# Layer two's first matrix product by Strassen's scheme, in a fused kernel of attention and two feed-forward layers

## Chip, cores and metric

The kernel runs on one core of one Trainium2 chip. The metric is the device time of one execution in microseconds, the median over runs; the profile is of one more execution of the same program.

## Reference

Attention over two batches of eight heads, 768 positions and 64 features each, in a window of 128 positions with four sink positions, then two feed-forward layers over the 1536 tokens of 512 features. The second layer, cut to what matters:

```python
n_tokens, d_model, d_ff = (1536, 512, 2048)

def _moe_ref(x, w_in, w_out):      # layer one
    h = x @ w_in
    g = np.maximum(0.01 * h, h)
    return (g @ w_out).astype(np.float32)

def _moe2_ref(x, w_in, w_out):     # layer two
    h = x @ w_in
    g = h * (1.0 / (1.0 + np.exp(-h)))
    return (g @ w_out).astype(np.float32)
```

## The kernel before

Every float32 operand of a matmul is split into a high part (rounded by ScalarE's copy into the type fp32r) and a low part (VectorE's subtraction of the high part from the whole); each product is three passes, high by high, high by low, low by high (`PASSES`). In the layers, the 2048 hidden features are 16 slices of 128 (`FT`), the tokens three blocks of 512 (`NB`), and a step `F` is one slice of one block of one layer: 96 steps, `steps` at its head. A step is two parts on PE. `hidden` multiplies a slice of w_in (`win`, four pieces of 128x128 along the 512 input features) by the block of x into the bank `h_ps`: 4 x 3 matmuls 512 wide, L805. `project` multiplies the slice of w_out by the hidden activations `g` into the four banks `y_ps`: again 12, L831. In layer two g is the stationary operand, so that y comes out with tokens on the partitions.

Between them, ACT takes `h_ps` twice (`take_hidden`, L466 into `g_f32`, L468 into the high part of `g`), and DVE makes the low part (`low_g`, L608). PE does hidden(F + 1) before project(F), which gives them the length of one part. Slices of weights come by DMA from SP's queue (`load_w`, L256) into a ring of four raw slots (`w_raw`, w_in and w_out of a slice side by side), and are split by ACT and DVE (`high_win` L453, `low_win` L597, `high_wout` L459, `low_wout` L603) into eight slots, `KEPT`. The tables `win_in` and `wout_in` say at which step. Blocks go through the slices in alternating directions, and the last eight of a block stay for the next, so 64 splits serve 96 steps. At the end of a block, `evacuate` brings `y_ps` out: in layer one as high and low part straight into `x` (L476, L618), in layer two into `out_sb`, from where SP stores it.

Attention runs ahead of layer one and beside it: its ticks `a` are woven into the steps up to F = 33. POOL works for attention alone: low parts of q, k and v (L330, L336, L345), of the attention's output (`low_x`, L315), and small copies (L306, L359). All engines run a program written out by hand, each in its own order, and wait for each other by semaphores. The order of PE for the steps behind attention is:

```python
for F in range(LAST - FS, NSTEP):
    if F + 1 < NSTEP:
        hidden(F + 1, 0)
        hidden(F + 1, 1)
    project(F, 0)
    project(F, 1)
```

Of the kernel before, what the change touches and what calls it, by code (L numbers as in the profile page):

```python
# [1 line left out]

# [9 lines left out]
P = 128  # L12
# [4 lines left out]
def sink_window_attention_two_ffn(  # L17
# [23 lines left out]
    KEPT = 8  # L41
# [4 lines left out]
    steps = [(layer, b, FT - 1 - i if b % 2 else i) for layer in (0, 1) for b in range(NB) for i in range(FT)]  # L46
    NSTEP = len(steps)
    N_L0 = FT * NB
# [4 lines left out]
    for F, (layer, b, f) in enumerate(steps):  # L53
        if (layer, f) not in resident:
            slot, left = free.pop(0)
            resident[layer, f] = len(split_w)
            split_w.append((layer, f))
            split_slot.append(slot)
            slot_left.append(left)
            first_step.append(F)  # L60
        j = resident[layer, f]
        split_of.append(j)
        if F % FT < FT - KEPT or b == NB - 1:
            del resident[layer, f]
            free.append((split_slot[j], F))
    NSPLIT = len(split_w)

# [8 lines left out]
    for j, s in enumerate(first_step):  # L76
        was, was_out = at, at_out
        start, i = s - s % FT, s % FT
# [36 lines left out]
    with ExitStack() as ctx:  # L115
# [9 lines left out]
        w_raw = sb("w_raw", [P, RING, 2 * HD], F32)  # L125
        win = sb("win", [P, KEPT, 2, HD], F32R)
        wout = sb("wout", [P, KEPT, 2, HD], F32R)

        x = sb("x", [P, 2, C, TILES * P], F32R)
        g_f32 = sb("g_f32", [P, 2, BLK], F32)  # L130
        g = sb("g", [P, 2, 2, BLK], F32R)

        qk_raw = sb("qk_raw", [P, 2, H // 2, QW], F32)
        v_raw = sb("v_raw", [P, HD], F32)
# [22 lines left out]
        filler = sb("filler", [P, 2 * P], BF16)  # L157
        out_sb = qk_raw[:, :, :, :].rearrange("p a b c -> p (a b c)")[:, 0:TB * HD].rearrange(
# [22 lines left out]
        def tokens(F):  # L181
            b = steps[F][1]
            return slice(b * BLK, (b + 1) * BLK)

# [31 lines left out]
        y_high, y_ready = sem("y_high"), sem("y_ready")  # L216
# [23 lines left out]
        def _(sp):  # L240
# [52 lines left out]
        def _(pool):  # L293
# [93 lines left out]

            for u in range(LAST):
# [545 lines left out]
```

## Time and profile before

| | |
|---|---|
| median of 3 runs | 667.64 us (667.15 to 668.63) |
| the profiled execution's own time | 668.03 us |
| its span, first to last instruction | 666.1 us |
| PE / ACT / DVE / POOL busy in the span | 638.8 / 299.9 / 278.7 / 120.0 us |
| mean granted clock of TensorE | 0.992 |
| read from HBM | 49.55 MB |

Span and busy times are of one execution. PE's busy time is that of its matmuls, which overlap: one lasts 0.39 us and the next starts before its end, so what a matmul costs is read from the distance of two starts. PEld is the load of the stationary operand, beside it. A group's "idle before" is time in which its engine stood before its instructions, with what ended that.

### The profile page before, as it was taken

Reading aid. Unit: us, or ns where it says so; the run is one execution under the profiler, and the core shown is the slowest. Engines: PE = TensorE matmul, PEld = TensorE weight load, DVE = VectorE, ACT = ScalarE, POOL = GpSimd, SP = SyncE. Lnnn points to the kernel's source line nnn. Section 1 sums busy time; section 2 is a strip of 40 time slices with the busy share of each in tenths; the row PEclk is TensorE's granted clock in tenths of the full one; section 3 lists DMA queues with packets and bytes.
Section 4 is the critical chain, followed back from the end, with each engine's and each line's share of the span. In section 5 each row is a group of like instructions: output and inputs, shape, how many; then the busy total and the mean of one; then the engine's idle time right before and its main releaser. Section 6 shows DMA issues by size and latency. Waiting matters only on the chain.

```text
span 666.1 us, 9036 instructions
## 1 busy us (share of the span) xinstructions
PE 638.8 (96%) x3091; PEld 526.7 (79%) x3091; DVE 278.7 (42%) x646; ACT 299.9 (45%) x676; POOL 120.0 (18%) x165
## 2 busy tenths in 40 slices
PE   8886999999989999999999999999999999999997
PEld 4675787777868888887888888888888888888886
DVE  3897456555535655543222234333322222212222
ACT  4787556555545565543333344333323333223332
POOL 5786324232314333310000000000000000000000
PEclk8999999999989999999999999999999999999999
DMA  6565233433322123111011123223211212201201
GB/s 148 147 189 161 64 112 96 132 107 112 95 81 64 49 64 112 64 33 31 1 63 64 64 68 110 98 101 99 95 64 31 64 63 64 96 0 64 63 1 63
DMA packets 16941, 53.27 MB, mean 80 GB/s; under 512 B 2561, under 2 KB 2561, under 8 KB 16897
## 3 DMA queue, kind: packets, MB, share of 16 engines
q1 hardware_dynamic: 16512, 52.63, 25.7%
q8 instruction: 25, 0.41, 0.3%
q14 instruction: 20, 0.16, 0.1%
q10 hardware_dynamic: 384, 0.07, 0.1%
HBM read 49.55 MB, written 3.15 MB: 79 GB/s over the span
## 4 chain that ended last, share of the span: by engine, by line
PE 77%; issue 9%; DVE 5%; ACT 4%; POOL 3%; DMA 2%; SPq 0%; POOLq 0%; ACTq 0%; DVEq 0%
PE h_ps L805 37%; PE y_ps L831 33%; PE o_ps L771 2%; DMA qk_raw<-qk 2%; PE s_ps L726 1%; ACT prob L416 1%; PE t_ps L739 1%; DVE win L597 1%; DVE wout L603 1%; DVE att L591 1%; ACT wout L459 1%; POOL k_hl L336 1%; DVE g L608 1%; ACT q_st L427 1%; POOL x L315 1%
## 5 line engine op out<-in xcount | busy, mean ns | idle before, releaser
L805 PE MATMUL h_ps<-x,win 128*128 128x512 f32 x1152 | 284.4, 394 | 9.4 <-DVE win L597 5.2
L805 PEld LDWEIGHTS h_ps<-x,win 128*128 128x128 f32 x1152 | 214.0, 189 | 54.2 <-DVE win L597 6.8
L466 ACT ACTIVATE g_f<-h_ps 128x512 f32<-128x512 f32 x96 | 57.4, 598 | 269.8 <-PE h_ps L805 269.6
L831 PE MATMUL y_ps<-g,wout 128*128 128x512 f32 x576 | 146.5, 395 | 1.2 <-PE o_ps L771 1.2
L831 PE MATMUL y_ps<-wout,g 128*128 128x512 f32 x576 | 138.2, 390 | 0.0
L603 DVE TENSOR_TENSOR wout<-w_raw,wout 128x512 fp32r<-128x512 f32 x64 | 46.7, 729 | 192.0 <-ACT wout L459 192.0
L831 PEld LDWEIGHTS y_ps<-wout,g 128*128 128x128 f32 x576 | 108.2, 188 | 22.4
L831 PEld LDWEIGHTS y_ps<-g,wout 128*128 128x128 f32 x576 | 104.0, 188 | 20.6 <-issue 1.9
L608 DVE TENSOR_TENSOR g<-g_f,g 128x512 fp32r<-128x512 f32 x96 | 66.1, 689 | 99.4 <-ACT g L468 99.4
L416 ACT ACTIVATE prob<-sm,neg_max 128x260 f32<-128x260 f32 (+1 forms) x96 | 47.0, 490 | 52.7 <-DVE neg_max L546 52.6
L468 ACT ACTIVATE g<-h_ps 128x512 fp32r<-128x512 f32 x96 | 57.0, 593 | 0.0
L597 DVE TENSOR_TENSOR win<-w_raw,win 128x512 fp32r<-128x512 f32 x64 | 49.1, 767 | 2.3 <-ACT win L453 2.3
L546 DVE CUSTOM_DVE_ANT_0 sm<-s_ps,mask 128x260 f32<-128x260 f32 (+1 forms) x71 | 28.7, 405 | 41.8 <-PE s_ps L726 41.1
L459 ACT ACTIVATE wout<-w_raw 128x512 fp32r<-128x512 f32 x64 | 40.4, 631 | 0.0
L453 ACT ACTIVATE win<-w_raw 128x512 fp32r<-128x512 f32 x64 | 40.3, 630 | 0.0
L330 POOL TENSOR_TENSOR q_st<-qk_raw,q_st 64x512 fp32r<-64x512 f32 x24 | 31.5, 1312 | 41.8 <-ACT q_st L427 40.2
L345 POOL TENSOR_TENSOR v_hl<-v_raw,v_hl 128x256 fp32r<-128x256 f32 x24 | 20.0, 834 | 100.6 <-ACT v_hl L435 100.5
L726 PEld LDWEIGHTS s_ps<-k_hl,q_st 128*128 128x128 f32 x142 | 26.9, 195 | 11.9 <-issue 3.5
L726 PE MATMUL s_ps<-k_hl,q_st 128*128 128x260 f32 (+1 forms) x142 | 30.2, 295 | 5.1 <-DVE neg_max L546 4.0
L771 PE MATMUL o_ps<-pT,v_hl 128*128 128x256 f32 x222 | 34.3, 288 | 0.1
L336 POOL TENSOR_TENSOR k_hl<-qk_raw,k_hl 128x528 fp32r<-128x528 f32 x22 | 31.1, 1413 | 1.7
L771 PEld LDWEIGHTS o_ps<-pT,v_hl 128*128 128x128 f32 x222 | 29.7, 191 | 0.7 <-DVE pT L554 0.4
(76 smaller groups left out, 407.4 us busy)
## 6 DMA issues: line engine op xcount, KB each, us to landing
w_raw<-w SPq DMA_DIRECT2D x64, 512.0 KB, 3.3
qk_raw<-qk SPq DMA_DIRECT2D x48, 260.0 KB, 4.4
v_raw<-vt SPq DMA_DIRECT2D x12, 256.0 KB, 3.7
y<-qk_raw SPq DMA_DIRECT2D x12, 256.0 KB, 2.3
vs_raw<-vsink ACTq DMA_DIRECT2D x8, 8.0 KB, 4.3
```

The lines of the kernel that those rows point to most:

```text
L416: nc.scalar.activation(prob[:, n % PR, 0:W], sm[:, n % 2, 0:W], ACT.Exp, scale=-1.0, bias=neg_max[:, n % 4:n % 4 + 1], accum_out=row_sum[: ...
L453: nc.scalar.activation(win[:, split_slot[j], 0, :], w_raw[:, j % RING, 0:HD], ACT.Copy).then_inc(win_high, 1)
L459: nc.scalar.activation(wout[:, split_slot[j], 0, :], w_raw[:, j % RING, HD:2 * HD], ACT.Copy).then_inc(wout_high, 1)
L466: nc.scalar.activation(g_f32[:, F % 2, :], h_ps[:, :], func, alpha=slope)
L468: nc.scalar.activation(g[:, 0, F % 2, :], h_ps[:, :], func, alpha=slope).then_inc(h_taken, 1)
L597: nc.vector.tensor_tensor(win[:, slot, 1, :], w_raw[:, j % RING, 0:HD], win[:, slot, 0, :].bitcast(F32), ALU.subtract).then_inc(win_ready, 1)
L603: nc.vector.tensor_tensor(wout[:, slot, 1, :], w_raw[:, j % RING, HD:2 * HD], wout[:, slot, 0, :].bitcast(F32), ALU.subtract).then_inc(wou ...
L608: nc.vector.tensor_tensor(g[:, 1, F % 2, :], g_f32[:, F % 2, :], g[:, 0, F % 2, :].bitcast(F32), ALU.subtract).then_inc(g_ready, 1)
L726: ins = mm(bank_[:, 0:W], q_st[:, h, :], k_hl[:, part, h, 0:W], start=part == HI, stop=part == LO)
L771: ins = mm(pair_out(u), v_hl[:, s, vp, p * P:(p + 1) * P], pT[:, u % 2, pp, s * 2 * P:(s + 1) * 2 * P], start=(u % 2 == 0 and s == 0 and v ...
L805: ins = mm(h_ps[:, :], win[:, split_slot[split_of[F]], wp, c * P:(c + 1) * P], x[:, xp, c, tokens(F)], start=(c == 0 and wp == HI and xp = ...
L831: ins = mm(y_ps[d][:, :], a[:, d * P:(d + 1) * P], r, start=(first and wp == HI and gp == HI), stop=(last and wp == LO))
```

## The change

Steps are now layer one's alone (48). Layer two goes by 24 pairs `q` of slices, eight for each block. For a pair, the product is cut into 2x2 parts in three ways: the two slices of hidden features, two halves of the 512 input features, two halves (256 tokens) of the block. Strassen's scheme makes the four quarters of the result of seven products instead of eight. Each product is two pieces of 128 along the features by three passes, so 6 matmuls of 256 columns, 42 for the pair, where hidden had 24 of 512 columns.

- Operands: five of the seven are sums or differences of quarters. POOL makes those of the weights (`sum_weights`, four operations per pair) and of layer one's output (`sum_x`, five per block); ACT and DVE split all seven (`high_w7`, `low_w7`; `high_xs`, `low_xs`). The weights' sums are made anew for every pair of every block; all 48 slices are loaded.
- Results: the scheme is arranged so that the two quarters off the diagonal grow in the two halves of one bank (`h_ps` and `s_ps` in turn), with one product in `t_ps`. After phase 0, DVE adds the halves (`shared`, a reduction) and subtracts that from `t_ps` (`e_sum`); after phase 1 ACT takes the quarters off the diagonal (`take_cross`), and PE goes on in the same bank; after phase 2, DVE adds `e_sum` (`sum_diagonal`, into `c_sum`), and ACT takes the diagonal from there (`take_diagonal`).
- `project_pair` has the 24 matmuls 512 wide of two steps, in two halves.
- Layer one's output stays whole as `y_f32` (one operation per bank instead of two). New buffers lie over those of attention and layer one. `KEPT` is 6, and layer one loads and splits 36 slices. The last steps of layer one prepare the first block's sums and the first two pairs' weights.

```diff
-    KEPT = 8
+    KEPT = 6
...
+    TAIL = NSTEP - 4
+    X_TICK = NSTEP - 14
...
-        elif i < FT - KEPT:
-            at = at_out = s - 6
         else:
-            i -= FT - KEPT
-            at = start + 2 + i + i // 2
-            at_out = at + 1
+            at, at_out = s - 4, s - 3
...
             def load_w(j):
                 layer, f = split_w[j]
-                wait(sp, win_ready, j - RING + 1)
+                if j < N_ONE + RING:
+                    wait(sp, win_ready, j - RING + 1)
+                else:
+                    q = (j - RING - N_ONE) // 2
+                    sp.wait_ge(w_sum, 4 * (q + 1))
+                    sp.wait_ge(w7_ready, 3 * q + 1)
                 wait(sp, wout_ready, j - RING + 1)
...
+            def sum_weights(q):
+                j = N_ONE + 2 * q
+                for i in range(2):
+                    pool.wait_ge(w_loaded[(j + i) % RING], 16 * ((j + i) // RING + 1))
+                if q > 1:
+                    pool.wait_ge(w7_ready, 3 * (q - 1))
...
+                nc.gpsimd.tensor_tensor(to[:, A11_A12:A11_A12 + 2, :], raw[:, :, 0, :], raw[:, :, 1, :],
+                                        ALU.add).then_inc(w_sum, 1)
+                nc.gpsimd.tensor_tensor(to[:, A21_A11, :], two[:, 1, :], one[:, 0, :],
+                                        ALU.subtract).then_inc(w_sum, 1)
...
+            for q in range(NPF):
+                if q + 2 < NPF:
+                    sum_weights(q + 2)
+                b, i = divmod(q, FP)
+                if b + 1 < NB and i < 7:
+                    sum_x(b + 1, i)
...
+            def low_w7(q):
+                j = N_ONE + 2 * q
+                dve.wait_ge(w7_high, 3 * q + 1)
+                nc.vector.tensor_tensor(w_part(q, A11, 2, 1), w_raw[:, j % RING:j % RING + 2, 0:2 * P],
+                                        w_part(q, A11, 2, 0).bitcast(F32), ALU.subtract).then_inc(w7_ready, 1)
+                for step, (i, n) in enumerate(((A11_A12, 2), (A21_A11, 3))):
...
+            def shared(q):
+
+                dve.wait_ge(m_done, 3 * q + 1)
+                xy = xy_bank(q)
+                nc.vector.tensor_reduce(d_sum[:, :], xy[:, :].rearrange("p (i n) -> p n i", i=2), mybir.AxisListType.X,
+                                        ALU.add).then_inc(d_ready, 1)
+                dve.wait_ge(d_ready, q + 1)
+                nc.vector.tensor_tensor(e_sum[:, :], z_ps[:, 0:2 * P], d_sum[:, :], ALU.subtract).then_inc(e_ready, 1)
...
+            def low_pair_g(q, half):
+                dve.wait_ge((a_taken, b_taken)[half], q + 1)
...
             evacuate(NSTEP - 1, 1)
+            for q in range(NPF):
+                store_half(q - 1, 1)
+                sum_diagonal(q)
+                low_pair_g(q, 1)
+                if q + 1 < NPF:
+                    shared(q + 1)
+                if q + 2 < NPF:
+                    low_w7(q + 2)
+                b, i = divmod(q, FP)
+                if b + 1 < NB and i < 7:
+                    low_xs(b + 1, i)
+                if q + 1 < NPF:
+                    low_pair_g(q + 1, 0)
+                if q + 2 < NPF:
+                    for i in range(2):
+                        low_wout(N_ONE + 2 * (q + 2) + i)
+                store_half(q, 0)
...
+            def product(q, w_i, x_i, to, start, stop=False):
+                for c in range(2):
+                    for wp, xp in PASSES:
+                        ins = mm(to, w_part(q, w_i, 1, wp)[:, 0, c * P:(c + 1) * P], x_part(q // FP, x_i, xp)[:, c, :],
+                                 start=start and c == 0 and wp == HI and xp == HI, stop=stop and c == 1 and wp == LO,
+                                 skip_group_check=True)
...
+            def strassen(q, phase):
...
+                if phase == 0:
+                    pe.wait_ge(w7_ready, 3 * (q + 1))
...
+                    product(q, A11_A22, B11_B22, z_ps[:, 0:2 * P], True, True)
+                    product(q, A11_A12, B22, c12, True)
+                    ins = product(q, A22_A21, B11, c21, False)
+                elif phase == 1:
+                    pe.wait_ge(e_ready, q + 1)
+                    product(q, A11, B12_B22, c12, False)
+                    ins = product(q, A22, B21_B11, c21, False)
+                else:
+                    pe.wait_ge(a_taken, q + 1)
+                    product(q, A21_A11, B11_B12, c12, False, True)
+                    ins = product(q, A12_A22, B21_B22, c21, False, True)
+                ins.then_inc(m_done, 1)
...
+            strassen(0, 0)
+            project(NSTEP - 1, 0)
+            strassen(0, 1)
+            project(NSTEP - 1, 1)
+            strassen(0, 2)
+            for q in range(NPF):
+                if q + 1 < NPF:
+                    strassen(q + 1, 0)
+                project_pair(q, False)
+                if q + 1 < NPF:
+                    strassen(q + 1, 1)
+                project_pair(q, True)
+                if q + 1 < NPF:
+                    strassen(q + 1, 2)
```

ACT's order per pair mirrors DVE's: `take_diagonal(q)`, `high_w7(q + 2)`, `high_xs`, `take_cross(q + 1)`, two `high_wout`.

How this stands on the engines. PE in layer two, before; a hidden part and a project part are each a dozen:

```order
L831 MATMUL y_ps<-wout,g 128x512 x12
L805 MATMUL h_ps<-x,win 128x512 x12
L831 MATMUL y_ps<-wout,g 128x512 x12
L805 MATMUL h_ps<-x,win 128x512 x12
L831 MATMUL y_ps<-wout,g 128x512 x12
```

and with the change, one pair (`g_50` is g2, `w_odd` the seven weight operands):

```order
L1090 MATMUL t_ps<-xs_even,w_odd 128x256 x6
L1090 MATMUL s_ps<-xs_even,w_odd 128x256 x12
L1137 MATMUL y_ps<-wout,g_50 128x512 x12
L1090 MATMUL s_ps<-xs_even,w_odd 128x256 x12
L1137 MATMUL y_ps<-wout,g_50 128x512 x12
L1090 MATMUL s_ps<-xs_even,w_odd 128x256 x12
```

Between the halves of the second product stand three phases of 18, 12 and 12 narrow matmuls, where two dozens of wide ones stood.

DVE in layer two, before, two steps with splits of weights:

```order
L597 TENSOR_TENSOR win<-w_raw,win 128x512
L603 TENSOR_TENSOR wout<-w_raw,wout 128x512
L608 TENSOR_TENSOR g<-g_f,g 128x512
L597 TENSOR_TENSOR win<-w_raw,win 128x512
L603 TENSOR_TENSOR wout<-w_raw,wout 128x512
L608 TENSOR_TENSOR g<-g_f,g 128x512 x2
```

and with the change, one pair:

```order
L839 TENSOR_TENSOR c_sum<-s_ps,e_sum 128x512
L846 TENSOR_TENSOR g_50<-g_f,g_50 128x512
L830 TENSOR_REDUCE d_sum<-h_ps 128x256
L833 TENSOR_TENSOR e_sum<-t_ps,d_sum 128x256
L814 TENSOR_TENSOR w_even<-w_raw,w_even 128x512
L818 TENSOR_TENSOR w_even<-w_sums,w_even 128x512
L818 TENSOR_TENSOR w_even<-w_sums,w_even 128x768
L824 TENSOR_TENSOR xs_even<-x_sums,xs_even 128x512
L846 TENSOR_TENSOR g_50<-g_f,g_50 128x512
L796 TENSOR_TENSOR wout<-w_raw,wout 128x512 x2
```

Two to six operations in two steps became eleven in a pair, and phase 1 of PE waits for the fourth.

POOL's program ended with attention before:

```order
L306 COPY inv_wide<-row_inv 128x256
L359 COPY prob_sink<-prob 128x4x8
L315 TENSOR_TENSOR x<-att,x 128x2x128 x2
L115 UNCONDITIONAL_BRANCH
```

and goes on in layer two now, five operations in each of the first pairs of a block:

```order
L471 TENSOR_TENSOR w_sums<-w_raw 128x512
L473 TENSOR_TENSOR w_sums<-w_raw 128x256
L475 TENSOR_TENSOR w_sums<-w_raw 128x256
L477 TENSOR_TENSOR w_sums<-w_raw 128x256
L493 TENSOR_TENSOR x_sums<-y_f_49 128x512
```

All five read two tensors in SBUF, as do eight of the eleven above.

## Rows read from the trace of the kernel before

**Rows 1.** The page: busy us (share) x instructions by engine; GB/s in 40 slices.

```profile
PE 638.8 (96%) x3091; PEld 526.7 (79%) x3091; DVE 278.7 (42%) x646; ACT 299.9 (45%) x676; POOL 120.0 (18%) x165
...
GB/s 148 147 189 161 64 112 96 132 107 112 95 81 64 49 64 112 64 33 31 1 63 64 64 68 110 98 101 99 95 64 31 64 63 64 96 0 64 63 1 63
```

**Rows 2.** Busy time by stretch, from block three of layer one on.

```profile
core 0: us, PE busy (x) PEld busy (x) DVE busy (x) ACT busy (x) POOL busy (x), PEclk, DMA share, GB/s
350.00:500.00 150.00, 150.00 (x663) 124.30 (x662) 48.26 (x76) 56.98 (x106) 0.00 (x0) 1.00 0.25 85
500.00:650.00 150.00, 150.00 (x663) 124.34 (x662) 39.33 (x61) 46.73 (x88) 0.00 (x0) 1.00 0.15 50
```

**Rows 3.** Timeline of PE, layer two: start, us, instructions, count.

```profile
536.95 2.88 PE L831 MATMUL y_ps<-wout,g 128*128 128x512 f32 x12
539.67 2.88 PE L805 MATMUL h_ps<-x,win 128*128 128x512 f32 x12
542.39 2.88 PE L831 MATMUL y_ps<-wout,g 128*128 128x512 f32 x12
```

**Rows 4.** Timeline, ACT and DVE of one step; in brackets the idle time before.

```profile
542.59 0.60 ACT L466 ACTIVATE g_f<-h_ps 128x512 f32<-128x512 f32 x1 [3.84 <-PE h_ps L805]
543.08 0.59 ACT L468 ACTIVATE g<-h_ps 128x512 fp32r<-128x512 f32 x1
543.56 0.63 ACT L459 ACTIVATE wout<-w_raw 128x512 fp32r<-128x512 f32 x1
544.08 0.63 ACT L453 ACTIVATE win<-w_raw 128x512 fp32r<-128x512 f32 x1
544.22 0.69 DVE L603 TENSOR_TENSOR wout<-w_raw,wout 128x512 fp32r<-128x512 f32 x1 [4.66 <-ACT wout L459]
544.83 0.69 DVE L608 TENSOR_TENSOR g<-g_f,g 128x512 fp32r<-128x512 f32 x1
...
545.43 0.69 DVE L597 TENSOR_TENSOR win<-w_raw,win 128x512 fp32r<-128x512 f32 x1
```

**Rows 5.** PE's 256-wide matmuls: a stretch of the timeline; durations min/median/max from 232 us.

```profile
232.82 0.88 PE L771 MATMUL o_ps<-pT,v_hl 128*128 128x256 f32 x6
233.54 1.53 PE L831 MATMUL y_ps<-g,wout 128*128 128x512 f32 x6
...
L771 PE MATMUL o_ps<-pT,v_hl x6: 278/282/286, 232.8 to 233.4; 128*128 128x256 f32 x6
```

**Rows 6.** Groups of DVE: busy us, mean ns | idle before.

```profile
L591 DVE TENSOR_TENSOR att<-o_ps,scale 64x256 f32<-64x256 f32 x40 | 16.8, 419 | 0.8 <-PE o_ps L788 0.5
...
L580 DVE TENSOR_REDUCE sum_eps<-row_sum 128x4 f32<-128x8 f32 x24 | 3.6, 151 | 0.0
...
L635 DVE TENSOR_REDUCE block_of<-ident 128x8 f32<-128x128 f32 x1 | 0.3, 256 | 0.0
```

**Rows 7.** Timeline of POOL, operations that nothing holds up.

```profile
174.07 0.74 POOL L315 TENSOR_TENSOR x<-att,x 128x256 fp32r<-128x256 f32 x1 [1.30 <-ACT x L447]
175.03 1.29 POOL L330 TENSOR_TENSOR q_st<-qk_raw,q_st 64x512 fp32r<-64x512 f32 x1 [0.22 <-POOL x L315]
176.40 1.32 POOL L336 TENSOR_TENSOR k_hl<-qk_raw,k_hl 128x528 fp32r<-128x528 f32 x1
```

**Rows 8.** Timeline of DVE and POOL where they meet.

```profile
228.35 1.80 DVE L597 TENSOR_TENSOR win<-w_raw,win 128x512 fp32r<-128x512 f32 x1
230.07 0.68 DVE L554 TENSOR_TENSOR pT<-t_ps,pT 128x512 fp32r<-128x512 f32 x1
...
228.31 1.29 POOL L330 TENSOR_TENSOR q_st<-qk_raw,q_st 64x512 fp32r<-64x512 f32 x1 [3.58 <-ACT q_st L427]
229.67 1.65 POOL L336 TENSOR_TENSOR k_hl<-qk_raw,k_hl 128x528 fp32r<-128x528 f32 x1
```

**Rows 9.** Loads of w_raw, issue to landing: from 330 us; and 60 to 320.

```profile
DMA to landing us min/median/max: 3.2/3.3/3.8
...
DMA to landing us min/median/max: 3.1/3.4/5.3
```

**Rows 10.** PE behind its longest wait: timeline, and its stretch in the windows.

```profile
190.39 4.43 PE L805 MATMUL h_ps<-x,win 128*128 128x512 f32 x12 [2.64 <-POOL x L315]
...
190.40:194.20 3.80, 3.80 (x12) 2.99 (x13) 0.00 (x0) 0.00 (x0) 0.00 (x0) 0.65 0.30 72
```

More of the change, by code:

```diff
@@ L1 @@
 from contextlib import ExitStack
+from math import prod
 import concourse.bass as bass
@@ L473, in evacuate @@
                 act.wait_ge((y_half, y_done)[half], F + 1)
-                for d in (2 * half, 2 * half + 1):
-                    if F < N_L0:
-                        nc.scalar.activation(x[:, 0, d, tokens(F)], y_ps[d][:, :], ACT.Copy).then_inc(y_high, 1)
-                    elif d % 2 == 0:
-                        wait(act, out_stored[d], 16 * steps[F][1])
-                        nc.scalar.activation(out_sb[:, d, :], y_ps[d][:, :], ACT.Copy).then_inc(out_act, 1)
+                d = 2 * half
@@ new lines, in evacuate, with high_w7 @@
+                nc.scalar.activation(y_f32[:, d, tokens(F)], y_ps[d][:, :],
+                                     ACT.Copy).then_inc(y_act, 1)
+            def high_w7(q):
+                j = N_ONE + 2 * q
+                for i in range(2):
+                    act.wait_ge(w_loaded[(j + i) % RING], 16 * ((j + i) // RING + 1))
+                if q == 1:
+                    act.wait_ge(x_ready, NHALF)
+                elif q > 1:
+                    act.wait_ge(m_done, 3 * (q - 1))
+                nc.scalar.activation(w_part(q, A11, 2, 0), w_raw[:, j % RING:j % RING + 2, 0:2 * P],
+                                     ACT.Copy).then_inc(w7_high, 1)
+                for i, n, sums in ((A11_A12, 2, 1), (A21_A11, 3, 4)):
+                    act.wait_ge(w_sum, 4 * q + sums)
+                    nc.scalar.activation(w_part(q, i, n, 0), w_sums[:, q % 2, i:i + n, :],
+                                         ACT.Copy).then_inc(w7_high, 1)
@@ new lines, in take_diagonal @@
+            def take_diagonal(q):
+                act.wait_ge(c_ready, q + 1)
+                if q:
+                    act.wait_ge(gp_ready, 2 * q)
+                else:
+                    act.wait_ge(g_ready, NSTEP)
+                src = c_sum[:, :, :].rearrange("p i n -> p (i n)")
+                nc.scalar.activation(g_f32[:, 1, :], src, ACT.Silu)
+                nc.scalar.activation(g2[:, q % 2, 0, 2:4, :].rearrange("p i n -> p (i n)"), src,
+                                     ACT.Silu).then_inc(b_taken, 1)
@@ L481, in _, with store_half @@
+            def store_half(q, half):
+                if q < 0 or q % FP != FP - 1:
+                    return
+                b, d = q // FP, 2 * half
+                act.wait_ge((y_half, y_done)[half], NSTEP + q + 1)
+                wait(act, out_stored[d], 16 * b)
+                nc.scalar.activation(out_sb[:, d, :], y_ps[d][:, :], ACT.Copy).then_inc(out_act, 1)
             for b in range(B):
@@ L792, in hidden @@
             def hidden(F, half):
-                layer, b, f = steps[F]
+                b, f = steps[F]
                 if half == 0:
@@ L822, in project @@
                 for d in (2 * half, 2 * half + 1):
-                    if first and blk:
-                        if blk <= NB:
-                            pe.wait_ge(y_ready, 4 * (blk - 1) + d + 1)
+                    if first and b:
+                        pe.wait_ge((y_act, y_dve)[d % 2], 2 * (b - 1) + d // 2 + 1)
+                    for wp, gp in PASSES:
+                        ins = mm(y_ps[d][:, :], wout[:, split_slot[split_of[F]], wp, d * P:(d + 1) * P],
+                                 g[:, gp, F % 2, :],
+                                 start=(first and wp == HI and gp == HI), stop=(last and wp == LO))
@@ new lines, in project_pair @@
+            def project_pair(q, diagonal):
+                b, i = divmod(q, FP)
+                pe.wait_ge(wout_ready, N_ONE + 2 * q + 2)
+                pe.wait_ge(gp_ready, 2 * q + 1 + diagonal)
+                first, last = i == 0 and not diagonal, i == FP - 1 and diagonal
+                for d in range(TB):
+                    s, at = ((0, 3), (0, 3), (1, 2), (1, 2))[d] if diagonal else ((1, 1), (1, 1), (0, 0), (0, 0))[d]
+                    if first:
+                        if b == 0:
+                            pe.wait_ge((y_act, y_dve)[d % 2], 2 * (NB - 1) + d // 2 + 1)
```

241 lines of the change are left out of this document (197 added, 44 removed).

## Prediction

> **What bounds the kernel now.** I read the page first: PE 96% busy, no other engine above 45% [rows 1]. The stretches then show where: between 350 and 650 us PE is busy all of 300 us at a granted clock of 1.00, and POOL does nothing [rows 2]. The timeline says what such a stretch is made of: twelve matmuls of L805, twelve of L831, each dozen starting 2.72 us after the last [rows 3]. So a 128x512 matmul costs 2.72/12 = 0.2267 us there, and a step of 24 costs 5.44 us; the 663 matmuls in each half of that stretch (0.226 us each) leave no room for a longer one. In the step shown, ACT waits 3.84 us for h_ps and DVE 4.66 us for ACT [rows 4]: they have room. The profiled run took 668.03 us around a span of 666.1, 0.4 us over the median of 667.64.
>
> **PE's own saving.** Of a pair of slices, 24 matmuls of 128x512 into h_ps go (24 x 0.2267 = 5.44 us) and 42 of 128x256 come; the 24 of the second product stay. What does a 256-wide one cost? Six of L771 last 0.88 us from first start to last end, one lasts 0.282 [rows 5], so they start (0.88 - 0.282)/5 = 0.120 apart; from the first of them to the next matmul is 233.54 - 232.82 = 0.72 us, again 0.120. I take 0.1195, between the first reading to four digits, 0.1196, and its rounding. Bounds: half of a 512-wide one, 0.1134, below; 0.125 above, twice the measured excess over that half. 42 x 0.1195 = 5.02 us, so a pair falls from 10.88 to 10.46 us, and 24 pairs save **10.1 us** (16.3 and 4.6 at the bounds). The upper bound is the whole eighth that the scheme saves in products; the rest goes for what each narrow matmul costs beside its columns. The Trainium skill (TensorE: Matmul & The Clock Gate, Back-to-back issue gap) gives N/2.4 + 2.5 ns, and an estimate by it is 215.8 and 109.2 ns and a saving of 24 x (24 x 215.8 - 42 x 109.2) ns = 14.2 us. By that rule the trace does not agree: the rows have 10 ns more on either width, and they decide.
>
> **What DVE gets.** Per pair, in program order: c_sum, low half of the diagonal g, the reduction, e_sum, three splits of w7 (512, 512, 768 elements), one split of a sum of y, low half of the cross g, two of wout. Starts of 512-wide operations in a row are 0.61 us apart, one lasts 0.685 [rows 4]; a 256-wide one from PSUM lasts 0.42 [rows 6], so 256 elements more are 0.27 and the 768-wide one takes 0.88 from start to start. The reduction I bound by [rows 6]: 151 ns for 8 elements and 256 for 128 make 0.59 for 512 by the slope, the other 512-wide operations 0.69; I take 0.68, since it reads PSUM. Between c_sum and the low half DVE has to wait for two Silus of ACT, 0.52 apart and 0.63 long [rows 4]: DVE stands 1.29 us. Sum: c_sum to low half 1.90, low half 0.61, reduction and e_sum with the wait between them 1.06, w7 2.10, y 0.61, cross 0.61, wout 1.22, together **8.1 us** against PE's 10.46. Alone it fits. e_sum would be there 0.8 us before PE wants it for phase 1.
>
> **What POOL gets, and where it collides.** POOL had no work in layer two [rows 2]; it now gets four sums of weights per pair (one of 512, three of 256), and in pairs 0 to 4 of the first two blocks a sum of y (512). Its operations of two SBUF inputs take 1.29 us for 512 and 0.74 for 256 [rows 7]. [rows 8] show what happens when such a one meets a DVE operation that also reads two SBUF tensors: at 228.31 POOL starts q_st, at 228.35 DVE starts the win split, which then takes 1.80 us for its 0.685 and ends 0.55 after POOL's; POOL's next one takes 1.65 for its 1.32, until DVE is done. They exclude each other for nearly their whole length. The pT split that starts at 230.07 reads PSUM and takes its 0.68 beside POOL's k_hl. The Trainium skill (SBUF — State Buffer, section SBUF: two separate sides) states it as an exclusive lock on a shared pair of ports, held for the whole instruction; the trace agrees by those 1.80 us. DVE so loses 1.80 - 0.69 = 1.11 us to a 512-wide POOL operation, 0.18 less than that takes; a 256-wide one costs 0.74 - 0.18 = 0.56.
>
> Do they meet? Eight of DVE's eleven (w7, y, both g, wout; c_sum, reduction and e_sum take an input from PSUM) are exposed, and each gives POOL the turn. POOL starts when the raw slices land. They are loaded when DVE has split the wout of the pair before in that slot, its last work ahead of c_sum: one load is issued about 0.5 us before c_sum starts, one 0.1 us after. A load alone lands in 3.3 us, beside others in up to 5.3 [rows 9]; I take 3.9 for the second, so POOL starts 4 us past the start of c_sum. DVE comes out of e_sum at 3.6, and into its exposed stretch. So all four sums of weights collide: 1.11 + 3 x 0.56 = 2.8 us, and DVE's pair takes 8.1 + 2.8 = **10.9 us**; with a sum of y 12.0 us. PE needs 10.46. The bound of layer two moves from PE to DVE in the first two blocks: per block five pairs lose 1.5, two 0.4, and the last, which has no split of y but two copies of y_ps (0.61 each), 1.0. That is 9.4 us, 18.9 for two, if nothing covers it. Laid out one after another from the start, the first two pairs of each block lose some 0.5 us instead of 3.0 (the 0.8 us ahead are used up first, and POOL's last sum falls into the time in which DVE waits for the Silus), so **14 us** of stalls are left (18.9 - 2 x 2.5), nearly all ahead of phase 1, by e_sum. In the third block there is no sum and no split of y: 10.3 us, PE bounds again.
>
> **The way in.** The last steps of layer one get w7 of the first two pairs. Behind hidden(47), DVE has the low g, three splits of w7, one of wout, then the first reduction, with POOL on the sums of pair 2 in between: e_sum comes 8.5 us after, PE wants it after projecting step 46 (2.72) and phase 0 (18 x 0.1195), and after projecting half of 47 (1.36), at 6.2. Stall **2.4 us**; without POOL about none. At the end the last diagonal half has less before it: 0.2 us.
>
> **Layer one.** Six slices kept instead of eight: 36 loads and splits instead of 32, two more in each of blocks 1 and 2 (ACT 2 x 0.52, DVE 2 x 0.61 each). In block 2 they have the room of [rows 4]. In block 1 they stand beside attention, where one win split met POOL [rows 8]; one or two more such meetings, each 1.1 us on DVE, cost PE perhaps a quarter. y now leaves PSUM by one operation per bank instead of two. I take **+0.5 us**, from -1.5 to +2.5. Silu's table load falls into idle time of ACT, as it did. 20 more loads of w_raw (84 for 64) make 1 MB per 10.9 us, about 96 GB/s, where 189 were reached [rows 1]: hidden.
>
> **Sum.** 668.0 - 10.1 + 14 + 2.4 + 0.2 + 0.5 = 675.0, and 0.4 less against the median: 674.6, which I take down to **674 us**, as the reduction by its slope would be 0.1 us a pair shorter, 1.0% slower.
>
> **Rivals.** (a) It goes as written on the other side: DVE's meetings with POOL stay within its 2.3 us of room (8.1 against 10.46). That takes 0.45 us per pair less than I count, or POOL starting 1.5 us later or 3 us earlier, in c_sum to e_sum, where DVE needs no second SBUF input. Then 10.1 us are saved, less 0 to 2.4 at the way in and 0.5: 657 to 660, or up to 666 if only the pairs with a sum of y stall (6 x 1.1 us). For it: nothing else is near a bound, and my excess is 4% of a pair. Against: the rows of the collision are plain, and the phase is set by the load. Chance 0.20. (b) Between the two, stalls of about 10 us: within 0.2% of 667.6; 0.08. (c) The reduction or the meetings cost more (0.3 us a pair over 18 pairs, +5), or the clock falls: a wait of 2.64 us for x was followed by twelve matmuls in 4.43 us instead of 2.88 [rows 10], a granted clock of 0.65; a few such in the stalls put the time at 679 to 684. 0.12, part of slower. (d) Narrow matmuls cost 0.125: +6 us on PE, but then PE hides 0.25 us a pair of the stalls; 676 to 678. 0.05. (e) That the forecast holds by its mechanism, 668.9 to 679: 0.55. The second product or the number of matmuls could not fail to change: the order shows 42 for 24.
>
> **Range and chances.** 0.2% is 1.3 us, about what a measurement here can tell. Slower: (c), (d), (e), 0.72; same 0.08; faster 0.20. The range leaves out the full gain of (a) and the worst of (c): 664 to 681.
>
> **What would show it.** After: 1008 matmuls of 128x256 in the products at 0.119 to 0.120 us; PE stretches in the third block still full, with pairs of 10.46 us; in the first two blocks idle PE of 4 to 12%, waited for by DVE's e_sum; DVE's splits of w7 and wout at means well above 0.69 us, c_sum at 0.69; POOL at work 3.5 to 4.8 us a pair, and longer where DVE holds it up. It is wrong if those splits stay at 0.69, if e_sum is not what PE waits for, or if pairs take 10.46 throughout.

## The result, and the profile after

| | before | after |
|---|---|---|
| median | 667.86 us (666.42 to 669.95, 7 runs) | 670.70 us (669.58 to 673.81, 7 runs) |
| ratio, 95% interval | | 1.0043 (1.0025 to 1.006) |
| the profiled execution, and its span | 668.03, 666.1 us | 673.81, 671.9 us |
| PE / DVE / POOL busy | [rows 1] | 636.5 / 431.7 / 265.8 us |

Slower, by 2.8 us: 0.43%. The forecast was 674.0, which is 6.4 over the 667.64 known then. The direction and the mechanism held; the size was over twice too large. The profiled execution of the change is its slowest, so stretches are compared here by their own lengths, and the end to end by medians.

The page of the kernel after, and its stretches in layer two (busy us and instructions of each engine, then PE's granted clock, DMA share, GB/s):

```profile
PE 636.5 (95%) x3523; PEld 538.7 (80%) x3523; DVE 431.7 (64%) x797; ACT 347.8 (52%) x755; POOL 265.8 (40%) x276
...
L471 POOL TENSOR_TENSOR w_sums<-w_raw 128x512 f32<-128x512 f32 x24 | 37.9, 1580 | 152.6 <-issue 106.7
```

```profile
400.00:490.00 90.00, 85.03 (x523) 75.20 (x522) 77.49 (x87) 43.42 (x77) 49.51 (x37) 0.98 0.24 82
490.00:577.00 87.00, 84.57 (x518) 73.99 (x517) 76.13 (x88) 45.17 (x81) 49.17 (x37) 1.00 0.33 109
577.00:650.00 73.00, 72.94 (x456) 65.33 (x455) 57.67 (x75) 36.47 (x65) 30.30 (x25) 1.00 0.31 102
```

The three stretches are roughly the three blocks of layer two. [rows 2] had PE busy throughout; now it stands 4.97 us in the first block (2.09 of it on the way in), 2.43 in the second, 0.06 in the third, where there are no sums of `y` to make or to split. POOL, idle before, works 49 of 90 us. What ends PE's idle time is in the view of waits (us in all, times, longest), from 398 to 640 us:

```profile
PE h_ps L1090 <- DVE e_sum L833: 4.3, 3, 2.1
PE s_ps L1090 <- DVE e_sum L833: 2.8, 3, 1.1
```

Nothing but `e_sum` is waited for. DVE's groups in the stretch from 400 to 640 us show what held it up (busy us, mean ns of one, idle before):

```profile
L796 DVE TENSOR_TENSOR wout<-w_raw,wout 128x512 fp32r<-128x512 f32 x43 | 47.3, 1135 | 0.0
L846 DVE TENSOR_TENSOR g<-g_f,g 128x512 fp32r<-128x512 f32 x43 | 39.9, 928 | 34.4 <-ACT g L640 25.6 <-ACT g L628 8.8
L818 DVE TENSOR_TENSOR w_even<-w_sums,w_even 128x512 fp32r<-128x512 f32 (+1 forms) x22 | 28.1, 1315 | 0.0
L833 DVE TENSOR_TENSOR e_sum<-t_ps,d_sum 128x256 f32<-128x256 f32 x22 | 9.3, 424 | 0.8
...
L830 DVE TENSOR_REDUCE d_sum<-h_ps 128x256 f32<-128x512 f32 x11 | 7.5, 684 | 0.0
...
L839 DVE TENSOR_TENSOR c_sum<-h_ps,e_sum 128x512 f32<-128x512 f32 x11 | 7.5, 680 | 0.5 <-PE h_ps L1090 0.4
```

The operations with an input in PSUM (the reduction, `e_sum`, `c_sum`) take what they take alone, 0.68 and 0.42 us. Those with two inputs in SBUF, 0.69 us each in [rows 4], average 0.93 (the low halves of g, L846) and 1.14 (the splits of wout, L796). So some of DVE's operations are stretched, besides the load that it has. One pair in the timeline, DVE and POOL interleaved (start, us, engine, line, operation, count; in brackets idle before):

```profile
458.00 0.68 DVE L839 TENSOR_TENSOR c_sum<-h_ps,e_sum 128x512 f32<-128x512 f32 x1
...
461.23 0.42 DVE L833 TENSOR_TENSOR e_sum<-t_ps,d_sum 128x256 f32<-128x256 f32 x1
461.57 0.68 DVE L814 TENSOR_TENSOR w_even<-w_raw,w_even 128x512 fp32r<-128x512 f32 x1
461.71 1.70 PE L1090 MATMUL s_ps<-xs_even,w_odd 128*128 128x256 f32 x12 [1.10 <-DVE e_sum L833]
462.17 2.65 DVE L818 TENSOR_TENSOR w_even<-w_sums,w_even 128x512 fp32r<-128x512 f32 x2
462.67 1.33 POOL L471 TENSOR_TENSOR w_sums<-w_raw 128x512 f32<-128x512 f32 x1 [5.14 <-issue]
463.96 1.46 POOL L473 TENSOR_TENSOR w_sums<-w_raw 128x256 f32<-128x256 f32 x1
464.74 1.23 DVE L824 TENSOR_TENSOR xs_odd<-x_sums,xs_odd 128x512 fp32r<-128x512 f32 x1
465.38 1.18 POOL L475 TENSOR_TENSOR w_sums<-w_raw 128x256 f32<-128x256 f32 x1
465.89 1.22 DVE L846 TENSOR_TENSOR g<-g_f,g 128x512 fp32r<-128x512 f32 x1
466.52 1.18 POOL L477 TENSOR_TENSOR w_sums<-w_raw 128x256 f32<-128x256 f32 x1
467.03 1.82 DVE L796 TENSOR_TENSOR wout<-w_raw,wout 128x512 fp32r<-128x512 f32 x2
468.78 0.68 DVE L839 TENSOR_TENSOR c_sum<-s_ps,e_sum 128x512 f32<-128x512 f32 x1
```

A POOL operation of 256 elements costs the DVE operation that it meets 0.54 us (1.23 for 0.69) and takes 1.18 itself for its 0.74. The pair, `c_sum` to `c_sum`, takes 10.78 us, with no sum of `y` in it. PE needs less: without a stall a pair is 10.50 to 10.52 us from start to start. The 1.10 in the bracket is what the pair before had run over: it had a sum of `y` and took 11.9.

**Where the stalls are.** From the first pair's start to the second's is 11.72 us, where 7.96 would do; from the second's to the last pair's 240.35, where 22 x 10.52 = 231.4 would do. So the way in costs 3.8 us and the loop 9.0. That is more than the waits listed: a pair of 10.78 us loses 0.26, which PE's modelled ends cover, so distances of starts are what to go by. From the start of layer two on PE to the end of the span the profiles have 267.9 us before (398.2 to 666.1) and 272.4 after (399.6 to 671.9): 4.5 us more.

### The profile page after: what moved, and what is told of

Same layout as the page of the kernel before. It is cut to its first block, busy times and chain, and to the rows that moved or that the text cites. A ratio compares the mean times of both kernels' runs of the same rounds, so it can differ in the third digit from the quotient of the medians.

```text
span 671.9 us, 10335 instructions
## 1 busy us (share of the span) xinstructions
PE 636.5 (95%) x3523; PEld 538.7 (80%) x3523; DVE 431.7 (64%) x797; ACT 347.8 (52%) x755; POOL 265.8 (40%) x276
## 4 chain that ended last, share of the span: by engine, by line
PE 62%; DVE 18%; issue 10%; ACT 5%; POOL 3%; ACTq 1%; DMA 1%; SPq 0%; POOLq 0%; DVEq 0%
PE h_ps L1062 17%; PE y_ps L1137 13%; PE y_ps L1082 13%; PE h_ps L1090 5%; PE s_ps L1090 5%; DVE wout L796 4%; PE o_ps L1030 2%; DVE g L846 2%; DVE w_odd L818 2%; PE t_ps L1090 1%; PE t_ps L998 1%; PE s_ps L985 1%; DVE w_even L818 1%; DVE win L790 1%; ACT prob L533 1%
## 5 line engine op out<-in xcount | busy, mean ns | idle before, releaser
L1062 PE MATMUL h_ps<-x,win 128*128 128x512 f32 x576 | 146.0, 398 | 9.5 <-DVE win L790 5.3
L1062 PEld LDWEIGHTS h_ps<-x,win 128*128 128x128 f32 x576 | 105.8, 190 | 32.1 <-DVE win L790 6.9
L796 DVE TENSOR_TENSOR wout<-w_raw,wout 128x512 fp32r<-128x512 f32 x84 | 79.5, 966 | 72.0 <-ACT wout L576 72.0
L471 POOL TENSOR_TENSOR w_sums<-w_raw 128x512 f32<-128x512 f32 x24 | 37.9, 1580 | 152.6 <-issue 106.7
L582 ACT ACTIVATE g_f<-h_ps 128x512 f32<-128x512 f32 x48 | 28.7, 597 | 92.6 <-PE h_ps L1062 92.5
L846 DVE TENSOR_TENSOR g<-g_f,g 128x512 fp32r<-128x512 f32 x48 | 43.3, 903 | 43.6 <-ACT g L640 29.3
L639 ACT ACTIVATE g_f<-c_sum 128x512 f32<-128x512 f32 x24 | 15.2, 632 | 87.7 <-DVE c_sum L839 87.7
L1090 PE MATMUL h_ps<-xs_even,w_even 128*128 128x256 f32 x288 | 39.1, 286 | 3.3 <-DVE e_sum L833 3.2
L1090 PEld LDWEIGHTS h_ps<-xs_even,w_even 128*128 128x128 f32 x288 | 37.2, 190 | 6.0 <-DVE e_sum L833 4.9
L1090 PEld LDWEIGHTS s_ps<-xs_even,w_odd 128*128 128x128 f32 x288 | 36.9, 191 | 4.4 <-DVE e_sum L833 3.4
L1090 PE MATMUL s_ps<-xs_even,w_odd 128*128 128x256 f32 x288 | 38.7, 284 | 1.8 <-DVE e_sum L833 1.7
```

The source lines that it names most:

```text
L471: nc.gpsimd.tensor_tensor(to[:, A11_A12:A11_A12 + 2, :], raw[:, :, 0, :], raw[:, :, 1, :], ALU.add).then_inc(w_sum, 1)
L796: nc.vector.tensor_tensor(wout[:, slot, 1, :], w_raw[:, j % RING, HD:2 * HD], wout[:, slot, 0, :].bitcast(F32), ALU.subtract).then_inc(wou ...
L846: nc.vector.tensor_tensor(g2[:, q % 2, 1, part, :], g_f32[:, half, :].rearrange("p (i n) -> p i n", i=2), g2[:, q % 2, 0, part, :].bitcast ...
L1062: ins = mm(h_ps[:, :], win[:, split_slot[split_of[F]], wp, c * P:(c + 1) * P], x[:, xp, c, tokens(F)], start=(c == 0 and wp == HI and xp = ...
L1090: ins = mm(to, w_part(q, w_i, 1, wp)[:, 0, c * P:(c + 1) * P], x_part(q // FP, x_i, xp)[:, c, :], start=start and c == 0 and wp == HI and ...
```

## Experiments

**The theory**: POOL's sums hold up DVE's operations of two SBUF inputs, DVE gets late with `e_sum`, and PE waits. (A meeting, below, is an operation of POOL and one of DVE, each with two inputs in SBUF, that are due at the same time; as in [rows 8], one then lasts until the other is done.) **The rivals**: (B) DVE is late by its own new work, (C) the loads or POOL's length are what is late. (D) came later: the number of POOL's operations in a pair counts, not when POOL starts them.

Each kernel is the changed one with the edit shown, except the last. "Way in" is the first pair's start on PE to the second's, "loop" the second's to the last's, both from the profiled run. The kernel before measured 667.94 to 668.06 beside them.

| run | median us | ratio, 95% | way in | loop |
|---|---|---|---|---|
| the change again | 671.70 | 1.0067 (1.0043 to 1.009) | 11.71 | 239.15 |
| sums on POOL one column wide | 659.87 | 0.9884 (0.9868 to 0.9899) | 7.96 | 231.39 |
| POOL gated | 659.47 | 0.9871 (0.9855 to 0.9888) | 7.97 | 231.39 |
| sums on DVE | 660.76 | 0.9891 (0.9873 to 0.9908) | 7.96 | 231.38 |
| sums of y gated | 665.26 | 0.9964 (0.995 to 0.9979) | 10.19 | 233.74 |
| first gate only | 671.01 | 1.0044 (1.0027 to 1.0061) | 7.97 | 242.36 |
| gated, more work on POOL | 659.60 | 0.9874 (0.9854 to 0.9894) | 7.95 | 231.40 |
| start late | 665.57 | 0.9954 (0.9935 to 0.9973) | 11.69 | 234.53 |
| start early | 673.50 | 1.0088 (1.006 to 1.0117) | 10.21 | 242.60 |
| before, six slices kept | 667.65 | 0.9996 (0.9985 to 1.0008) | | |

**The change again**, unchanged, for a second profile.

> The changed kernel once more, to part what it costs from what one profiled execution adds. Both theories: 670.7 us again (669.6 to 673.8). If the 3 us by which the first profiled execution lay above the median came from the clock falling behind the 2.09 us wait at the way into layer two, then a profile with a span near 668 has a granted clock of 1.00 in the 10 us behind that wait, and one near 672 has not. The stalls by e_sum in pairs 1 to 17 are 9 to 10 us in either.

The median came at 671.70, 1.0 over the first series. The guess about the clock was wrong: behind the wait on the way in PE ran at half rate in both profiles, here for the last of twelve narrow matmuls and for six wide ones (granted clock 0.81 and 0.50 in these two rows):

```profile
402.27 2.08 PE L1090 MATMUL h_ps<-xs_even,w_even 128*128 128x256 f32 x12 [2.09 <-DVE e_sum L833]
404.15 2.76 PE L1082 MATMUL y_ps<-g,wout 128*128 128x512 f32 x6
```

Where it did not fall ("sums of y gated", below) the same rows are 1.69 and 1.56, so the fall costs 0.39 + 1.20 = 1.6 us here. Of the 4.2 us between the two profiled spans 1.2 are in the loop and 3.1 ahead of layer two, which starts at 396.5 us here and at 399.6 in the first profile. The clock fell there in the first and not in this one: 0.57 at 54.5 to 58.5 us (1.00 before and here), 0.79 at 188 to 196 (1.00 here).

**Take POOL's work away.** The sums (from pair 2 on, and those of `y` for the second and third block) are made one column wide: their values are left out, and only their instructions stay.

```diff
+                if q > 1:
+                    to, raw = to[:, :, 0:1], raw[:, :, :, 0:1]
+                    one, two = raw[:, 0, :, :], raw[:, 1, :, :]
...
+                n = 1 if b else 2 * P
+                nc.gpsimd.tensor_tensor(x_sums[:, i % 2, :, 0:n], y_part(b, k0, n0)[:, :, 0:n],
+                                        y_part(b, k1, n1)[:, :, 0:n], op).then_inc(xs_sum, 1)
```

> POOL's sums for pairs 2 to 23 and for the second and third block cut to one column (their values are left out, every instruction and every wait stays). Theory A, the meetings of POOL and DVE: no PE wait for e_sum is left, all pairs 10.50 us, DVE's splits of w7 and wout at 0.69 us; 670.7 - 9.4 (pairs) - 2.1 (way in) = 659 us, 658 to 660.5. Theory B, DVE has too much of its own work or the reduction is slow: stalls stay, 668 to 671. Theory C, the 20 more loads and when they land: stays as well, 668 to 671.

659.87 us: 8.1 below before. Every stall is gone. Its group of `wout` splits from 400 to 640 us, against 1135 ns above:

```profile
L801 DVE TENSOR_TENSOR wout<-w_raw,wout 128x512 fp32r<-128x512 f32 x46 | 29.7, 685 | 0.0
```

**Move POOL's work in time.** All the work is kept; POOL waits until PE has ended phase 2 of the pair, which is when DVE's `c_sum` begins.

```diff
                     pool.wait_ge(w7_ready, 3 * (q - 1))
+                    pool.wait_ge(m_done, 3 * (q - 1))
```

> One more wait on POOL: sum_weights(q), q from 2, waits for m_done 3(q - 1), the same event that releases c_sum. POOL's sums of a pair then run while DVE makes c_sum, waits for the Silus and reduces, where it needs no second SBUF input, and they still come before ACT's split of them. The amount of work on every engine is unchanged. Theory A: nearly all stalls go, those of the way in too (the sums of pair 2 come behind it); pairs 10.50 us, 659 us, 658 to 662, faster than both kernels. Theory B or C: a wait more can only delay, 671 to 675.

659.47 us: one wait more, and the kernel is 1.3% faster than before and 11 to 12 us (1.7 to 1.8%) faster than the change as written. That speaks against (B) and (C): nothing of DVE's work or of the loads is less, and POOL's first sum now waits for PE and not for a load. Its stretches, for the same windows as above, and two pieces of its timeline:

```profile
400.00:490.00 90.00, 90.00 (x567) 81.20 (x566) 66.28 (x96) 49.80 (x87) 38.83 (x37) 1.00 0.27 94
490.00:577.00 87.00, 87.00 (x553) 79.02 (x553) 65.50 (x93) 47.65 (x84) 40.70 (x39) 1.00 0.33 119
```

```profile
459.67 0.69 DVE L840 TENSOR_TENSOR c_sum<-s_ps,e_sum 128x512 f32<-128x512 f32 x1 [1.00 <-PE s_ps L1091]
459.81 1.30 POOL L472 TENSOR_TENSOR w_sums<-w_raw 128x512 f32<-128x512 f32 x1 [4.96 <-PE s_ps L1091]
461.06 0.74 POOL L474 TENSOR_TENSOR w_sums<-w_raw 128x256 f32<-128x256 f32 x1
461.58 0.77 DVE L847 TENSOR_TENSOR g<-g_f,g 128x512 fp32r<-128x512 f32 x1 [1.22 <-ACT g L641]
461.75 1.20 POOL L476 TENSOR_TENSOR w_sums<-w_raw 128x256 f32<-128x256 f32 x1
462.27 0.68 DVE L831 TENSOR_REDUCE d_sum<-h_ps 128x256 f32<-128x512 f32 x1
462.91 0.74 POOL L478 TENSOR_TENSOR w_sums<-w_raw 128x256 f32<-128x256 f32 x1
462.99 0.42 DVE L834 TENSOR_TENSOR e_sum<-t_ps,d_sum 128x256 f32<-128x256 f32 x1
```

POOL now works in the 3.65 us from `c_sum` to `e_sum`, in which DVE reads PSUM or waits for the Silu. Beside those, its operations take their undisturbed 1.30 and 0.74 us; the third meets the one split that lies there, and takes 1.20, the split 0.77 for 0.69. DVE waits 1.00 us for PE before `c_sum`: PE bounds again.

**The sums on DVE itself.** The same four sums, and those of `y`, as DVE operations behind `e_sum`; POOL's loop over the pairs is gone:

```diff
+                if q + 2 < NPF:
+                    sum_weights(q + 2)
+                if b + 1 < NB and i < 7:
+                    sum_x(b + 1, i)
                 if q + 2 < NPF:
                     low_w7(q + 2)
```

> The weights' sums from pair 2 and the sums of y for blocks two and three move from POOL to DVE, behind e_sum: 1.6 us more work per pair on DVE (0.61 + 3 x 0.34), with a sum of y 2.2, and no POOL in layer two. Theory A: DVE needs 8.1 + 1.6 = 9.7 us of 10.50, in ten pairs 10.3; few stalls, 659 to 663 us though DVE has more to do. Theory B: DVE's load is the bound, so 2 us more of it per pair cost 10 us or more, above 680. Theory C: 670 to 672.

660.76 us, no stall in the loop, with 1.6 us more of DVE's own work per pair: (B) falls. A sum takes it 0.68 (512) or 0.42 us (256), starting 0.60 and 0.34 apart, so four make 0.60 + 3 x 0.34 = 1.6 us. On POOL, at the wrong moment, they cost DVE 2.8.

**Price the sum of y alone.**

```diff
+                if b:
+                    pool.wait_ge(c_ready, FP * (b - 1) + i + 1)
```

> Only POOL's sums of y for blocks two and three wait, for c_sum of the running pair (c_ready), so that each runs while DVE stands for the two Silus. The weights' sums stay as in the changed kernel. This prices the one term that decides the size of the miss: the pairs in which the sum of y meets DVE. In the two profiles of the changed kernel 5 and 4 pairs took 11.6 to 11.9 us. Theory A: they fall to 10.8, 5 x 1.1 = 5.5 us less or a little more, stalls in the loop fall from 9 to 3 or 4 us, the way in stays: 665 us, 663.5 to 667. If the sums of the weights alone make the stalls, nothing changes: 671.

The loop shrinks to 233.74 and the median by 5.4 us (6.4 against the change run again). The meetings of the sum of `y` were some 70% of the loop's loss (6.6 of 9.0 us, 5.4 of 7.8 in the second profile); the sums of weights alone leave 2.3. The way in shrank too, to 10.19, as the clock did not fall there in this profile; the 2.09 us of waiting stayed. In how many of the other executions it fell is not known, so the loop prices the sum of `y` better than the median does.

**Gate the first sums only**, for the way in.

```diff
+                if q == 2:
+                    pool.wait_ge(m_done, 3)
```

> Only the weights' sums of pair 2 wait, until phase 2 of pair 0 is done; they no longer meet DVE at the way into layer two. Theory A: the wait of 2.1 us ahead of phase 1 of pair 0 goes, and the half clock behind it, which made the first interval 3.76 us longer than without sums; up to 2 us come back in pair 2, whose splits wait for the later sums. 667 to 669.5 us. If the clock falls there for another reason, only the 2.1 us go.

A miss: the way in fell to 7.97 as expected, but the median stayed at 671.01, outside the 667 to 669.5 expected. The gain came back as a loss in the loop, 242.36. The sums that were held up ran into the next ones: POOL worked without a gap from 405.48 to 417.68, with two sums of `y` in one pair, both where DVE has splits to do:

```profile
409.27 1.29 POOL L495 TENSOR_TENSOR x_sums<-y_f 128x512 f32<-128x512 f32 x1
...
415.94 1.74 POOL L495 TENSOR_TENSOR x_sums<-y_f 128x512 f32<-128x512 f32 x1
```

That pair took 12.76 us, and the last of the first block 11.37. Against the two profiles of the change the loop lost 2.0 and 3.2 of the 3.7 us gained: here the stall was mostly moved, by the wait that removed it, into a loop in which DVE had no room for it.

**More work for POOL, in the right place.** The gated kernel, with one 256-wide sum made twice per pair:

```diff
                 nc.gpsimd.tensor_tensor(to[:, A11_A22, :], one[:, 0, :], two[:, 0, :],
+                                        ALU.add).then_inc(again, 1)
+                pool.wait_ge(again, q + 1)
+                nc.gpsimd.tensor_tensor(to[:, A11_A22, :], one[:, 0, :], two[:, 0, :],
                                         ALU.add).then_inc(w_sum, 1)
```

> The gated kernel with one more 128x256 sum per pair on POOL (the last one made twice, behind a wait of POOL for itself), so 0.74 us more work and 0.2 us more waiting on POOL per pair. Theory A: what counts is when POOL uses the SBUF inputs, not how much it does; the added sum ends about where DVE comes out of e_sum, and DVE has 2 us to spare in a pair: 659.5 us, 658 to 661. A bound by POOL's amount of work would cost 0.9 x 22 = 20 us.

659.60 us: no change, and what was left of (C) falls. Neither POOL's length nor the number of its operations bounds the gated kernel; what counts is when they run.

**Why the loss was smaller than forecast.** In both profiles of the change, pairs with a sum of `y` take either 11.8 to 11.9 or 10.8 to 10.9 us. The second pair (`c_sum` 1 to 2) took 11.89 in one execution, with POOL starting 4.23 us past `c_sum`, and 10.80 in the other, with 5.05. Two kernels keep that start from coming before a given moment, by making the sums of weights wait for one or two of DVE's splits of w7 as well:

```diff
-                    pool.wait_ge(w7_ready, 3 * (q - 1))
+                    pool.wait_ge(w7_ready, 3 * (q - 1) + (2 if q > 2 else 0))
```

with 2 for "start late" and 1 for "start early".

> From pair 3 on POOL's sums of weights also wait for DVE's second split of w7 of the pair before, which ends 4.85 us past c_sum: POOL starts at 4.9 us or later, never at 3.6 to 4.7. Theory: the phase of POOL's start decides whether the sum of y costs anything; started at 4.9 or later it falls past the next c_sum, into DVE's wait for the Silus. So no pair of the first two blocks is longer than 10.85 us, first pair's start to last pair's start takes 236 us (240.35 and 239.15 in the two profiles of the change), and the median is 667 us, with e_sum waited for by 0.3 us a pair. Rival (the number of operations decides, wherever they start, as I summed it): pairs with a sum of y stay at 11.9, 239 to 241, 671.

> The same gate one split earlier: POOL starts at 4.3 us past c_sum or later. Theory: between 3.6 and 4.7 all starts are alike, so this changes nothing but by chance: pairs with a sum of y at 11.9 wherever the load has landed by 4.7 (four to seven of ten), 239 to 241.5 from first to last pair, 670 to 672. If a gate as such did something, or any delay helped in proportion, this one would give a good part of what e9 gives.

Start late, from the second `c_sum` to the third, POOL and then DVE:

```profile
426.22 1.85 POOL L471 TENSOR_TENSOR w_sums<-w_raw 128x512 f32<-128x512 f32 x1 [3.80 <-DVE w_odd L818]
...
431.47 1.75 POOL L493 TENSOR_TENSOR x_sums<-y_f 128x512 f32<-128x512 f32 x1
```

```profile
429.69 2.38 DVE L796 TENSOR_TENSOR wout<-w_raw,wout 128x512 fp32r<-128x512 f32 x2
431.99 0.68 DVE L839 TENSOR_TENSOR c_sum<-h_ps,e_sum 128x512 f32<-128x512 f32 x1
```

Start early, the same:

```profile
425.78 1.58 POOL L471 TENSOR_TENSOR w_sums<-w_raw 128x512 f32<-128x512 f32 x1 [4.89 <-DMA w_raw<-w]
...
431.03 1.74 POOL L493 TENSOR_TENSOR x_sums<-y_f 128x512 f32<-128x512 f32 x1
```

```profile
430.39 2.92 DVE L796 TENSOR_TENSOR wout<-w_raw,wout 128x512 fp32r<-128x512 f32 x2
433.24 0.68 DVE L839 TENSOR_TENSOR c_sum<-h_ps,e_sum 128x512 f32<-128x512 f32 x1
```

POOL starts 5.03 us past `c_sum` (421.19) in the first and 4.42 past it (421.36) in the second. In the second the sum of `y` meets the two `wout` splits, which take 2.92 instead of 2.38. In the first it waits its turn until those are done and lies beside `c_sum` and the wait for the Silu. A start 0.6 us later makes the pair 10.80 us instead of 11.88, and the kernels differ by 7.9 us in the median. Late: no pair of the first two blocks over 10.84, loop 234.53 (236 expected: POOL's sums came later still in one pair, which took 10.45). Early: the six pairs with a sum of `y` that started at 4.4 to 4.5 took 11.9, two whose load landed after 5 us took 10.8, and the last of the first block 11.38. I had expected it to equal the change (670 to 672, loop 239 to 241.5); at 242.60 and 673.5 it is above that, as all four early pairs pay where the change had three, and the last pair of the first block pays 0.6. The two kernels have the same operations on every engine, so rival (D) falls.

**Layer one's part**, the kernel before with six slices kept:

```diff
-    KEPT = 8
+    KEPT = 6
...
+            at, at_out = s - 4, s - 3
```

> The kernel before with six slices kept and the change's rule for when they are split (w_in four steps ahead, w_out three), in both layers: 72 loads and splits instead of 64, layer two unchanged otherwise. What I counted at +0.5 us, from -1.5 to +2.5, by itself: 668.0 to 668.5 us. If six slices kept are what makes the changed kernel slower, it is 670 to 671.

667.65 us, -0.3 against before, within the interval of about 0.8 either way: eight more loads and splits (72 for 64, four of the eight in layer one) cost nothing that can be told.

## Why the forecast was right in direction and too large

Point by point, by its own steps:

- **PE's own saving: 10.1, measured 8.7.** A pair without a stall is 10.52 us from start to start in the gated kernel (231.39 / 22), not 10.46; 24 x (10.88 - 10.52) = 8.7. The narrow matmul was right: by the mean distances of starts in the gated kernel a pair's 42 take 5.02 us, as forecast. The 24 wide ones, which I left at 5.44, take 5.50: behind a change of width the first five start 0.229 to 0.235 us apart, the later ones 0.227 to 0.229. The Trainium skill (TensorE: Matmul & The Clock Gate, Back-to-back issue gap) gives N/2.4 + 2.5 ns for an isolated matmul, and says that for a stream of weight loads and matmuls it counts too much at a large N. The trace does not agree: 512-wide ones start 226.7 ns apart, 10.9 more than the rule has, and the saving was 8.7 and not the 14.2 of the estimate by it.
- **What DVE gets: held.** `e_sum` ends 3.65 us past `c_sum` (3.6 forecast), and a pair is 10.79 us with 2.76 of meetings in it (1.11 + 3 x 0.55, late start), so 8.03 alone (8.1). That is worked out and not seen: without the meetings PE sets the pair.
- **The meeting of POOL and DVE: held, in kind and price.** Forecast 1.11 and 0.56 us, measured 1.1 and 0.54; pairs of 10.9 and 12.0 forecast, 10.8 and 11.9 measured. Removing POOL's work, moving it in time and moving it to another engine all ended the stalls, and more of it in the harmless place did not bring them back. The Trainium skill (SBUF — State Buffer, section SBUF: two separate sides) states an exclusive lock, held for the whole instruction. The trace agrees: an operation that meets another ends later by the other's length less some 0.2 us.
- **The loop's stalls: 14 forecast, 9.0 and 7.8 in the two profiles. This step failed**, in "I take 3.9 for the second, so POOL starts 4 us past the start of `c_sum`", which set one start for all pairs. (The 9.4 of a block is 9.3 by its rounded terms, which changes nothing.) The view of the loads from 410 us gives issue to landing, against [rows 9]:

```profile
DMA to landing us min/median/max: 3.1/3.8/5.1
```

So POOL starts 3.4 to 5.5 us past `c_sum` (2.1 and 2.2 in the first pair), and the sum of `y` costs 1.1 us or nothing as that falls before or after some 4.8. The 14 had six pairs at the full 1.5, and some 5 for the others: the first two of each block, two more at 0.4, the boundary pair at 1.0. Measured in the first profile are five long pairs with 6.3 together and ten of 0.27 with 2.7; in the second, four with 5.1 and ten with 2.7. In the second block the first two paid in full, which I had thought covered, and the next three, charged in full, did not. The boundary pairs, charged 1.0, lost 0.3, as POOL's sum of `y` again falls past `c_sum`; started early, the first of them lost 0.9. I had seen the other side of this, "POOL starting 1.5 us later", as a rival for the whole kernel; for the sum of `y` alone 0.8 was enough, and it came pair by pair. Where the start is held early the loop loses 11.2 us (242.60 - 231.39), with two loads landing late even there; an estimate with these two at 1.1 as well is 13.4, near my 14. That this kernel's 673.5 is near my 674 is in part an offset: its loop is 2.8 below mine, PE's saving 1.4 short.
- **The way in: 2.4, measured 3.8.** The wait was right (2.09). Behind it the clock fell in both profiles of the change, for 1.6 us, which I had only as part of rival (c).
- **Layer one: +0.5, not told apart from nothing.** The slices kept are -0.3 +- 0.8. For layer one as a whole there is only the start of layer two in single executions: 398.2 us before, 396.5 to 400.5 in the ten profiles with the change (mean 398.8). The end, charged 0.2, is within 0.1 us of the gated kernel's.

In sum: -8.7 + 9.0 + 3.8 = 4.1 us with the first profile's loop and 2.9 with the second's (7.8). By the trace, from the start of layer two to the end of the span, it is 4.5 and 3.3, so 0.4 stays for the end and what is not named; the gated kernel has 259.7 us there for 267.9, 8.2 less, again 0.4 short of its 8.7. The medians have +2.8 and +3.8. The working errs by 5 to 6 us in the loop, offset by 1.4 each in PE's saving and on the way in. Of the signs that I named, idle PE of 4 to 12% in the first two blocks came in the first (5.5%) and not in the second (2.8%).

That the result is on the same side as the forecast is the mechanism's doing, but by a small margin, and in that partly luck: with POOL's start held at 5.0 us past `c_sum` or later it would have turned (665.6).

## What to carry to other kernels

- Work given to an idle POOL is not free if DVE has operations of two SBUF inputs at that time: each meeting cost DVE 0.2 us less than POOL's operation takes alone. Gate POOL by a semaphore into DVE's phases with PSUM inputs or waits; here one such wait was worth 11 to 12 us and made a change that lost 0.4% gain 1.3%.
- Where a loop's engines are within some per cent of each other, ask for the phase of the late engine's start in every iteration, not its mean: a load that lands 0.6 us later moved pairs from 11.9 to 10.8 us.
- A stall removed in front of a loop that is bound elsewhere can come back in it, here 2.0 to 3.2 us of 3.7: look at the loop again, and not at the stall alone.

## What was not expected of the hardware

- A later start made the kernel faster: with the same operations on every engine, 665.57 against 673.5 us. What differs is whether POOL's fifth operation meets DVE's splits of wout or lies beside `c_sum`.
- A wait of 2.09 us on PE was followed in three profiles (the change twice, start late) by half-rate matmuls at a cost of 1.6 us, and in two (sums of y gated, start early) by none, with the same wait. What tells these apart stays open.
- Loads of w_raw landed in up to 5.1 us in layer two, where they had 3.8 at most before (from 330 us on, [rows 9]), at a DMA share of only 0.33. Why was not tried.
